# Small steps moved between the places of a fused attention and mixture-of-experts kernel's three engine orders

## The reference

```python
# x [4,8,512,64], state [4,8,32,64]
scores = scale * x @ state^T;   xread = softmax(scores) @ state
scores2 = scale * state @ x^T;  sread = softmax(scores2) @ x
x = concat([xread, sread], axis=2) -> 2176 rows of 512
h = x @ w_in                        # 512 -> 2048
g = h * tanh(softplus(h))           # mish
y = g @ w_out                       # 2048 -> 512
# then: route each row of y to 1 of 8 experts (cosine similarity to emb, softmax gate),
# out = gate * (relu(y @ w1[e]) @ w2[e]),  512 -> 1024 -> 512
```

## Time and profile before

| | us |
|---|---|
| runs, median (lowest to highest) | 665.69 (665.31 to 667.47) |
| the profiled execution | 665.31 |
| its span, first to last instruction | 663.5 |
| PE busy | 643.5 (97%) |
| PE weight loads busy | 497.3 (75%) |
| DVE busy | 442.6 (67%) |
| ACT busy | 388.5 (59%) |

### The profile page before, as it was taken

The page is one execution under the profiler, slowest core; times in us unless marked ns, Lnnn a source line. Parts: engine busy times, 40 slices in busy tenths (PEclk is TensorE's granted clock), DMA queues, the critical chain, the costliest instruction groups (busy, mean ns, idle before and its releaser), DMA issues.

```text
span 663.5 us, 12455 instructions
## 1 busy us (share of the span) xinstructions
PE 643.5 (97%) x4174; PEld 497.3 (75%) x4175; DVE 442.6 (67%) x701; ACT 388.5 (59%) x501; POOL 53.0 (8%) x76
## 2 busy tenths in 40 slices
PE   7889999999999999999999999999999999999996
PEld 6667777677776677776668878788888888888884
DVE  7899999988788789775768668644521641271271
ACT  2789778796668686786877472533421631261260
POOL 2000000000300001100002121100100100100101
PEclk9989999999999999999999999999999999999999
DMA  8812547200433000534000622854501541163140
GB/s 253 255 34 99 190 128 213 73 1 2 132 126 125 3 1 17 177 109 146 0 2 33 251 84 93 279 185 134 200 32 48 174 146 48 48 207 126 48 158 6
DMA packets 35351, 72.73 MB, mean 110 GB/s; under 512 B 5699, under 2 KB 5699, under 8 KB 35312
## 3 DMA queue, kind: packets, MB, share of 16 engines
q1 hardware_dynamic: 27728, 56.93, 26.7%
q0 software_dynamic: 3040, 9.13, 3.5%
q10 hardware_dynamic: 4544, 6.14, 3.1%
HBM read 60.92 MB, written 12.16 MB: 110 GB/s over the span
## 4 chain that ended last, share of the span: by engine, by line
PE 75%; DVE 12%; ACT 6%; issue 3%; DMA 3%; ACTq 0%; POOL 0%; SPq 0%; DVEq 0%; POOLq 0%
PE PS L641 20%; PE PS L748 16%; PE PS L777 16%; PE PS L597 9%; PE PS L757 2%; PE PS L622 2%; PE PS L551 2%; PE PS L535 2%; PE PS L662 1%; DVE ww L1488 1%; ACT ww L1044 1%; DVE qq L1500 1%; DVE qq L1483 1%; PE PS L729 1%; PE PS L506 1%
## 5 line engine op out<-in xcount | busy, mean ns | idle before, releaser
L641 PE MATMUL PS<-WH,gh 128*128 128x512 f32 x256 | 104.4, 408 | 0.8 <-DVE gl L1506 0.8
L641 PE MATMUL PS<-WH,gl 128*128 128x512 f32 x256 | 101.1, 395 | 0.0
L641 PE MATMUL PS<-WL,gh 128*128 128x512 f32 x256 | 101.1, 395 | 0.0
L1144 ACT ACTIVATE hh<-PS 128x512 fp32r<-128x512 f32 x40 | 21.9, 596 | 91.4 <-PE PS L757 88.3
L1582 DVE TENSOR_TENSOR WL<-raw,WH 128x1024 f32 (+1 forms) x48 | 56.0, 1220 | 20.3 <-ACT WH L1124 19.2
L777 PE MATMUL PS<-WH,hh 128*128 (+1 forms) x160 | 65.3, 408 | 0.0
L777 PE MATMUL PS<-WH,hl 128*128 (+1 forms) x160 | 63.0, 394 | 0.0
L777 PE MATMUL PS<-WL,hh 128*128 (+1 forms) x160 | 62.9, 393 | 0.0
L641 PEld LDWEIGHTS PS<-WH,gh 128*128 128x128 f32 x256 | 48.4, 189 | 17.9 <-issue 6.7
L1601 DVE TENSOR_SCALAR osb<-PS,gid 128x512 f32<-128x512 f32 x21 | 15.7, 750 | 66.9 <-PE PS L777 66.9
L1124 ACT ACTIVATE WH<-raw 128x1024 f32 (+1 forms) x48 | 47.6, 1055 | 21.4 <-issue 7.5
(11 more groups left out here) (275 smaller groups left out, 1242.3 us busy)
## 6 DMA issues: line engine op xcount, KB each, us to landing
raw<-in_w SPq DMA_DIRECT2D x48, 512.0 KB, 3.3
raw<-in_w_in SPq DMA_DIRECT2D x36, 512.0 KB, 5.0
yg<-by_expert ACTq DMA_DIRECT2D x22, 260.0 KB
raw<-in_w_out SPq DMA_DIRECT2D x8, 512.0 KB, 6.0
by_expert<-junk SPq DMA_DIRECT2D x1, 2080.0 KB, 9.8
wr<-in_w_in SPq DMA_DIRECT2D x4, 512.0 KB, 9.2
x_0a<-in_x SPq DMA_DIRECT2D x8, 128.0 KB, 4.4
x_0b<-in_x SPq DMA_DIRECT2D x8, 128.0 KB, 4.9
```

Source lines behind the costliest of these rows:

```text
L641: mm = pe.matmul(PS[:, 2 + t, :], a[:, v % 2, e, t * P:t * P + P], w[:, 8 + p, e * 512:e * 512 + 512], start=(p == 0 and e == 0 and i == 0 ...
L1144: a.activation(hidden(end)[0][:, 4 * j:4 * j + 4, :], PS[:, 3 + j, :].rearrange("p (k m) -> p k m", k=4), ACT.Copy).then_inc(hh_rdy, 1)
```

## The change

It moves steps within the written orders of the three engines. Nothing is added or left out, no instruction changes, and no step is moved past a DMA issue.

- TensorE: score(1) from between the halves of Y(3) to behind Y(3); route_t(2, 0) from between the halves of Y of unit (3, 2) to ahead of it.
- ScalarE: sread_out(0) from behind mish_b and o_split of unit 6 to ahead of mish_b of unit 6, with exp_1(1) ahead of it; M_hi(1, 3) one unit later; y_out(0) behind the mish_b of its unit; turned(c, 1) and turned(c, 3) of batches 0 and 1 from ahead of mish_c to behind it.
- VectorE: sread_scale(0) from behind mish_lo to ahead of mish_g in unit 5; route_b of batches 0 and 1 ahead of the unit's mish_q, A_lo(2) and A_lo(3) to the unit's end; M_lo(1, 3) one unit later; y_out(0) from ahead of mish_e to behind mish_r; sread_scale(2) and (3) from ahead of mish_g to behind it.

```diff
--- before.py
+++ after.py
@@ -823,7 +823,6 @@
                     M(c + 1, p - 5)
                 if c == 3:
                     if p == 2:
-                        Y(v, (0,))
                         route_t(2, 0)
                     if p == 3:
                         route_l(2, 1)
@@ -839,10 +838,7 @@
                     if p == 7:
                         Y(v, (0,))
                         TY(t0)
-                if v == 3:
-                    Y(v, (0,))
-                    score(1)
-                Y(v, (1,) if v in (0, 3) or c in (1, 2) and p == 3 or c == 3 and p in (2, 4, 7) else (0, 1))
+                Y(v, (1,) if v == 0 or c in (1, 2) and p == 3 or c == 3 and p in (4, 7) else (0, 1))
                 if v < 2:
                     M(0, v + 2)
                 if c in (1, 2):
@@ -853,6 +849,8 @@
                         route_l(c - 1, 2)
                         route_t(c - 1, 3)
                 if c == 0:
+                    if p == 3:
+                        score(1)
                     if p == 4:
                         sread_turned(0)
                 if c < 3:
@@ -1162,7 +1160,6 @@
                 mish_b(u)
                 if u == 6:
                     o_split(6)
-                    sread_out(0)
                 if u < PC - 1:
                     mish_t(u + 1)
                 if u == 6:
@@ -1172,8 +1169,6 @@
                     o_split(7)
                     break
                 mish_w(u + 1)
-                if u == 5:
-                    exp_1(1)
                 if u == 6:
                     A_hi(1)
                 mish_hi(u)
@@ -1189,6 +1184,9 @@
                 if u == 4:
                     scores_out(1)
                     o_split(5)
+                if u == 5:
+                    exp_1(1)
+                    sread_out(0)
             for u in range(PC, len(SEQ)):
                 kind, c, p = SEQ[u]
                 n = p if kind == "m" else -1
@@ -1208,7 +1206,7 @@
                         turned(done, 2)
                     if n == 5 and c == 3:
                         turned(done, 2)
-                if kind == "m" and (n == 0 and c == 1 or n == 2 and c > 1):
+                if kind == "m" and (n in (0, 2) and c == 1 or n == 2 and c > 1):
                     M_hi(c, n + 1)
                 if c > 1 and n == 1:
                     sread_out(c)
@@ -1218,13 +1216,7 @@
                     exp_1(c + 1)
                 if n == 6 and c in (1, 2):
                     A_hi(c + 1)
-                if c == 1 and n == 1:
-                    y_out(done)
                 mish_b(u)
-                if c == 1 and n == 1:
-                    M_hi(1, 3)
-                if n in (3, 4) and 0 < c < 3:
-                    turned(done, (1, 3)[n - 3])
                 if (kind, p) == ("z", 1):
                     turned(2, 0)
                 if c == 3 and n == 4:
@@ -1235,9 +1227,10 @@
                     M_hi(c + 1, 0)
                 if n == 2 and c in (1, 2):
                     scores_out(c + 1)
-                if c > 1 and n == 1:
+                if done >= 0 and n == 1:
                     y_out(done)
-                    M_hi(c, 2)
+                    if c > 1:
+                        M_hi(c, 2)
                 mish_c(u)
                 if c == 1 and n == 0:
                     M_hi(1, 2)
@@ -1245,7 +1238,10 @@
                     if n == 2:
                         squares(done, (0, 1) if c < 3 else range(ST))
                     if n == 3 and c < 3:
+                        turned(done, 1)
                         squares(done, (2, 3))
+                    if n == 4 and c < 3:
+                        turned(done, 3)
                     if n == 5:
                         if c == 3:
                             turned(done, 3)
@@ -1675,6 +1671,8 @@
             for u in range(1, PC):
                 mish_e(u)
                 mish_r(u)
+                if u == 5:
+                    sread_scale(0)
                 if u == 6:
                     M_lo(1, 0)
                 mish_g(u)
@@ -1685,8 +1683,6 @@
                 if u == 6:
                     A_lo(1)
                 mish_lo(u)
-                if u == 5:
-                    sread_scale(0)
                 if u > 1:
                     o_rest(u)
                 if u == 1:
@@ -1709,19 +1705,16 @@
                 kind, c, p = SEQ[u]
                 n = p if kind == "m" else -1
                 done = c - 1 if kind == "m" else -1
-                if c == 3 and n == 7:
+                if done >= 0 and n == (7 if c == 3 else 6):
                     route_b(done)
                 mish_q(u)
                 if SEQ[u - 1][0] == "m":
                     mish_lo(u - 1)
-                if c in (1, 2) and n == 6:
-                    route_b(done)
-                    A_lo(c + 1)
                 if done >= 0 and n == (6 if c == 3 else 5):
                     route_a(done)
                 if n == 7 and c in (1, 2):
                     M_lo(c + 1, 1)
-                if kind == "m" and (n == 0 and c == 1 or n == 2 and c > 1):
+                if kind == "m" and (n in (0, 2) and c == 1 or n == 2 and c > 1):
                     M_lo(c, n + 1)
                 if c == 1 and n == 0:
                     soft_2(1)
@@ -1729,23 +1722,19 @@
                     soft_5(1)
                 if n == 4 and c in (1, 2):
                     soft_2(c + 1)
-                if c == 1 and n == 1:
-                    y_out(done)
                 mish_e(u)
                 mish_r(u)
                 if n == 6 and c in (1, 2):
                     M_lo(c + 1, 0)
                 if n == 1 and c > 1:
                     M_lo(c, 2)
-                if c > 1 and n == 1:
+                if done >= 0 and n == 1:
                     y_out(done)
+                mish_g(u)
                 if n == 0 and c > 1:
                     sread_scale(c)
-                mish_g(u)
                 if c == 1 and n == 0:
                     M_lo(1, 2)
-                if c == 1 and n == 1:
-                    M_lo(1, 3)
                 if c in (1, 2):
                     if n == 0:
                         turn_x(c + 1, 0)
@@ -1764,6 +1753,8 @@
                         sread_scale(1)
                     if n == 5 and c > 0:
                         soft_5(c + 1)
+                    if n == 6 and c > 0:
+                        A_lo(c + 1)
                 if c == 3 and n == 6:
                     lo_gz(0)
                 if c == 3 and n == 7:
```

## The result

The changed kernel takes 672.96 us (median of 4, 672.26 to 674.93) beside 666.27 for the kernel before (4 runs): 1.0105 times, with a 95% interval of 1.0081 to 1.013. Slower, as forecast, and 0.7 from the predicted 672.3. The profiled execution took 672.58, its span 670.8.

The account below looks back on a forecast made before the run. TensorE, busy for 97% of the span with its order nearly closed, was taken as the bound. The steps' lags summed to 6.85: 665.31 + 6.85 = 672.2 us profiled, 672.5 by the median, taken as 672.3; range 668.3 to 675.3.

Parts of the forecast that it names:

- 6: Batch 1's routing in batch 2's pass: turned copies behind mish_c delay route_l, no wait at route_s to win; +1.25 us.
- 7: route_b(1) ahead of mish_q(22): H(23) waits 1.25 for mish_q, the 0.40 wait of M(3, 0) goes; +0.85 us.
- 1: Unit 6, late score(1) and early sread_out(0): the queue behind sread_out, not VectorE's delay, makes H(8) late; +1.0 us.
- 2: y_out(0) behind mish_r(9) on VectorE: its copy ends later and Y(8) waits for it; +1.45 us.
- 3: M_lo(1, 3) one unit later: score(2), which writes its banks, waits for it; +0.27 us.
- 4: Batch 0's turned copies behind mish_c: route_l(0, 1) waits, +1.15, the wait at route_s goes, -0.45; +0.8 us in all.
- 5: route_b(0) ahead of mish_q(14), A_lo(2) ahead of mish_q(15): H(16) late, +0.45 us; sread_scale(2) behind mish_g, +0.2.
- 8. and 9.: sread_scale(3) behind mish_g delays sread_turned(3), +0.6 us; route_t(2, 0) ahead of Y of (3, 2), 0.
- rival of half speed: TensorE's clock falls once or more: 674.0 us for once, 675.7 for twice; chance 0.10.
- Partly covered: ScalarE and VectorE catch up faster, so the later waits shrink to a third: 668.3 to 670.3 us; chance 0.16.
- the rival on the other side: All moved steps reach TensorE in time and the waits taken away remain as gain: 663.3 to 665.3 us; chance 0.09.
- Only the first pass counts: Only steps 1 to 3 cost time, the routing copies being needed later: 668.0 us; chance 0.05.

Follow-up runs that it names:

- b_yout: The kernel before with only y_out(0) moved late, behind mish_r on VectorE and behind mish_b on ScalarE: 666.97 us, 1.0015.
- a_routeb: The changed kernel with route_b of batches 0 and 1 and A_lo(2), A_lo(3) put back behind mish_lo: 670.94 us, 1.0076.
- a_scale: The changed kernel with sread_scale(2) and (3) put back ahead of mish_g: 671.97 us, 1.0088.
- b_sread: The kernel before with only sread_out(0) moved ahead of mish_b(6) on ScalarE, and exp_1(1) behind mish_hi(5): 666.86 us, 1.0013.
- b_score: The kernel before with only score(1) moved behind Y(3) instead of between its halves: 666.69 us, 1.0013.
- a_yout: The changed kernel with y_out(0) alone put back to its old places on ScalarE and VectorE: 674.04 us, 1.0131.

## Why the prediction was right

The mechanism was right: TensorE's order is all but closed, and each moved step costs what it arrives late at its meeting. The steps' sum was 6.85 and the traces give 6.42 over the same meetings. That the time came out within 0.7 is in part luck: 0.9 of the difference of the spans lies outside the nine steps, and the errors of steps 6 and 7 cancel. By its own steps:

1. Place right, size nearly (1.0 against 0.83). mish_t(7) came 1.02 later, counted like the lag, but M_hi(1, 0) followed it by 0.91 instead of 1.09 and was only 0.84 late, and that went on to H(8). "What comes last there is another step" was half of it: score(1) alone makes H(8) 0.64 late, which that step had waved off.
2. and 3. Right to 0.03, and the chain is what sets them (b_yout). What the prediction did not see is that 2 shields 3: without it score(2) waits 2.21 and the clock falls.
4. The wait ahead of route_l and the return at route_s came as said; 0.2 too much, in the last small terms.
5. Right in its sum. The two terms belong together in one direction: without the wait at H(16), sread_turned(2) takes the whole 0.65 (a_routeb); without the one at sread_turned(2), H(16) stays nearly as it was, and 0.3 is won (a_scale).
6. and 7. Each is off by 0.34, in opposite directions; that they make 2.10 together, as predicted, is luck in the terms. Before, route_s of batch 1 had a small wait that overlapping records hid ("no wait ahead of route_s to win" was wrong); TensorE won 0.29 there and lost it at H(23), which waits for VectorE's time and not for TensorE's: the lag grew by 1.60 there where 1.25 was forecast. The 0.40 of M(3, 0) came (0.30), but not by route_b's move (a_routeb).
8. and 9. Right. The wait ahead of H(29) only moved, to route_t(2, 0), 0.92, and 0.17 stayed.

The rival of half speed did not come in the stretch of the moved steps (PEclk 1.00 from 68 to 334 us), where the new waits are 1.42 at the most; in the experiment with a wait of 2.21 it did. *Partly covered* and the rival on the other side fall: the lag never shrinks by more than the 0.64 that step 4 gives back at route_s and behind. *Only the first pass counts* falls too, as steps 4 to 8 took the lag from 2.58 to 6.42. The Trainium skill (TensorE: Matmul & The Clock Gate, Why this matters for your kernels) advises against gaps of TensorE longer than any named here. As a line below which the clock is safe, these traces don't bear it out: the gap of 2.21 was followed by half speed at once, and here the measurement decides.

Two figures of the prediction don't follow from its own terms. The bounds of the steps add up to 2 and 11, not to 3 and 9; and the first rival without step 4's 0.8 is 669.6, not 668.5. Neither moved the forecast. Its list of waits also leaves out 1.05 within sread(0) at 82.3 us, called "issue"; it is 1.01 in the changed kernel, so the change didn't touch it.

## What to carry to other kernels

Where one engine's order is nearly closed, walk along it and write down, for every place at which it takes something from another engine, when that arrives and what lies queued ahead of it; a moved step of 0.6 to 2 us costs the difference, and the sum of such differences held to half a us in seven. Prices of single moves don't add: two late steps that meet at one place cost one wait, and undoing one of a pair can bring out a longer wait behind it, so moves have to be undone, or tried, in the groups that meet. The other way round, the short list of waits of the kernel before was a list of gains that did add, for the two moves tried (1.10 and 1.63, together 2.63).

## What was not expected of the hardware

- Each fall of the clock in the thirteen traces, the end of the span left aside, is 3.4 us at half speed and goes with a wait of TensorE of 1.80 to 2.41 us: 17 in all, nine of them at the wait of 2.3 near 43 us, seven at waits of 1.80 to 2.41 in the first 24 us, and the one behind 2.21 ahead of score(2), which cost 1.77. It begins between half a us before the end of the wait and 1.4 behind it.
- The length of the wait doesn't decide it. Waits of 2.37 and 2.78 ahead of score(0) (b_sread, b_score) and of 2.90 ahead of H(0) (a_yout) were not followed by a fall, those of 1.96 to 2.02 ahead of score(0) were in four traces (the changed kernel's among them). What decides it stays open. So does why these four all belong to the six traces with the changed kernel's orders, which differ from the others' only from 66 us on.
- The wait near 43 us is followed by half speed in nine traces and not in four. In the changed kernel it was not; there H(5) waited 0.74 for mish_q a little later, a wait which the trace of the kernel before, where the clock had fallen, doesn't have (in the other three without the fall it is 0.73 to 0.75). So a part of what the clock costs is had back at the next meeting.
- One execution of 3278.69 us among some 160 of all kernels stays open. TensorE is busy in all of it at a granted clock recorded as 1.00, its products of line L641 taking 1.73 us where they take 0.41 in the changed kernel, while VectorE's and ScalarE's busy times (448 and 396) are within 3% of the usual.
